# Attention with cluster masks, a routed and a dense expert layer on one core: another order of the opening, of GpSimd's additions and of the seam between the two expert layers

## The reference

```python
# attention: 2 batches, 8 heads, 768 tokens, 64 wide; 16 centroids a head
q_assign = argmax(normed(q) @ normed(centroids).T)      # cluster of each query, the same for k
mask     = q_assign[..., :, None] == k_assign[..., None, :]
scores   = where(mask, (q @ k.T) / sqrt(64), -1e9)
x        = softmax(scores) @ v                          # -> x: 1536 tokens x 512
# routed experts: 8 experts, 512 -> 1024 -> 512, the best one for each token
expert   = argmax(normed(x) @ normed(expert_emb).T / tau)
x        = gate * (relu(x @ w1[expert]) @ w2[expert])   # gate: the softmax at that expert
# dense experts: 8 experts, all of them for each token
P        = exp(x @ w_gate - max)
for _ in range(8):                                      # rows, then columns, brought to a sum
    P /= P.sum(1) ; P /= P.sum(0) ; P *= 1536 / 8
out      = sum(P[:, e] * (relu(x @ w1[e]) @ w2[e]) for e in range(8))
```

## Time and profile before

| | us |
|---|---|
| median of 3 runs | 1592.2 (1591.24 to 1592.25) |
| the profiled execution, its own time | 1594.29 |
| its span in the trace | 1592.5 |
| TensorE busy | 1568.3 (98%) |
| VectorE busy | 1190.0 (75%) |
| ScalarE busy | 770.6 (48%) |
| GpSimd busy | 263.7 (17%) |

### The profile page before, as it was taken

One profiled execution on the slowest core, in us unless ns is written; L12 is line 12 of the kernel. 1 busy time (PEld: TensorE's weight loads), 2 busy tenths in 40 slices (PEclk: granted clock), 3 DMA queues, 4 the chain that ended last, 5 costly groups with the idle time before them and its releaser, 6 DMA issues.

```text
span 1592.5 us, 27473 instructions
## 1 busy us (share of the span) xinstructions
PE 1568.3 (98%) x8404; PEld 1390.7 (87%) x8404; DVE 1190.0 (75%) x2026; ACT 770.6 (48%) x1418; POOL 263.7 (17%) x343
## 2 busy tenths in 40 slices
PE   8999999999999999999999999999999999999998
PEld 7999999778888788989999898989899998989897
DVE  7999999999999976876656666666656566666664
ACT  5777779888888852323232323233232333232321
POOL 2111111342333550000100100010001001100102
PEclk9999999999999999999999999999999999999999
DMA  4222323354344310100110010011001100100002
GB/s 101 61 60 69 79 59 90 86 198 148 143 151 151 106 41 27 40 28 27 47 33 27 29 51 27 27 40 40 27 27 45 35 27 28 52 26 27 27 0 79
DMA packets 123701, 94.92 MB, mean 60 GB/s; under 512 B 66345, under 2 KB 101161, under 8 KB 123633
## 3 DMA queue, kind: packets, MB, share of 16 engines
q1 hardware_dynamic: 120848, 86.01, 17.8%
q0 software_dynamic: 2480, 8.13, 1.5%
q10 hardware_dynamic: 304, 0.05, 0.0%
HBM read 87.88 MB, written 6.29 MB: 59 GB/s over the span
## 4 chain that ended last, share of the span: by engine, by line
PE 88%; DVE 7%; issue 3%; ACT 2%; DVEq 0%; DMA 0%; ACTq 0%; POOL 0%
PE moe_bank L1381 11%; PE moe_bank L1383 11%; PE moe_bank L1382 11%; PE moe_bank L1356 10%; PE moe_bank L1359 10%; PE moe_bank L1358 10%; PE attn_ps_out L447 3%; PE attn_ps_probs_t L428 2%; PE moe_bank L1316 2%; PE moe_bank L1318 2%; PE moe_bank L1317 2%; PE moe_bank L1299 2%; PE moe_bank L1301 2%; PE moe_bank L1300 2%; DVE attn_scores L697 1%
## 5 line engine op out<-in xcount | busy, mean ns | idle before, releaser
L2035 DVE SCALAR_TENSOR_TENSOR all_x<-moe_bank,all_x 128x512 f32<-128x512 f32 x336 | 251.4, 749 | 130.8 <-PE moe_bank L1383 130.2
L1356 PE MATMUL moe_bank<-moe_x_t_hi,all_w_hi 128*128 128x384 f32 x896 | 303.0, 338 | 2.0 <-DVE all_w_lo L889 1.4
L1359 PE MATMUL moe_bank<-moe_x_t_hi,all_w_lo 128*128 128x384 f32 x896 | 302.5, 338 | 0.0
L1381 PE MATMUL moe_bank<-moe_w_hi,moe_h_hi 128*128 128x512 f32 x768 | 302.3, 394 | 0.0
L1358 PE MATMUL moe_bank<-moe_x_t_lo,all_w_hi 128*128 128x384 f32 x896 | 301.1, 336 | 0.0
L1382 PE MATMUL moe_bank<-moe_w_lo,moe_h_hi 128*128 128x512 f32 x768 | 300.5, 391 | 0.0
L1383 PE MATMUL moe_bank<-moe_w_hi,moe_h_lo 128*128 128x512 f32 x672 | 264.5, 394 | 0.0
L1356 PEld LDWEIGHTS moe_bank<-moe_x_t_hi,all_w_hi 128*128 128x128 f32 x896 | 168.4, 188 | 13.4 <-issue 2.0
L1358 PEld LDWEIGHTS moe_bank<-moe_x_t_lo,all_w_hi 128*128 128x128 f32 x896 | 168.4, 188 | 10.0
L1359 PEld LDWEIGHTS moe_bank<-moe_x_t_hi,all_w_lo 128*128 128x128 f32 x896 | 168.2, 188 | 0.0
L2196 POOL TENSOR_TENSOR moe_w_sums<-moe_dense_w_raw 128x256 f32<-128x256 f32 x32 | 24.8, 774 | 842.4 <-DVE all_w_lo L889 842.4
(11 more groups left out here) (339 smaller groups left out, 3071.4 us busy)
## 6 DMA issues: line engine op xcount, KB each, us to landing
...
moe_dense_w_raw<-in_moe_w SPq DMA_DIRECT2D x32, 512.0 KB, 3.4
...
```

What stands on the lines that cost most here:

```text
L1356: pe.matmul(out, hi[:, s, k, :], XH[chunk][:, x, k, :], start=(start and k == 0), stop=False, skip_group_check=True)
L1359: mm = pe.matmul(out, lo[:, s, k, :], XH[chunk][:, x, k, :], start=False, stop=(stop and k == 1), skip_group_check=True)
L1381: pe.matmul(out, HH[h][hidden][:, rows], W2H[j][:, f, :], start=(f == 0), stop=False)
L2035: dve.scalar_tensor_tensor(acc, y, PROB[:, row, bass.ds(at, 1)], acc, ALU.mult, ALU.add).then_inc(y_added, 1)
```

## The change

In the opening, `UnitRows` is now one object for the centroids and one for the embeddings, each with its own load, root and writes. The embeddings are squared and written by ScalarE, and made exact on VectorE behind the splits of head 0. k's first loads go through ScalarE's queue, the embeddings' and tau's through SP's. The centroids' splits stand ahead of those of the second and third thirds; head 0's similarities are computed by thirds, each when its third is split; the first block of scores and four fillers follow them, and the third block of scores now comes ahead of head 1's similarities and the embeddings' transposes. Head 1's third third is transposed behind the key ids and split behind the first two maxima.

In the items the row addition is two operations of 128x256, each of which waits until VectorE has split half of the next item's w2. The token sums of pairs 0, 1 and 2 stand behind the additions of items 13, 14 and 15, with a third buffer; all are GpSimd's. That buffer lies where the dense w1's second landing place is, so `load1(0, 1)` waits until pair 2 is transposed. In the last item VectorE splits the hidden rows ahead of w2's last two parts. In the first unit the sums and splits of the second weight part come earlier on all three engines (ahead of pair 4's sums on GpSimd), and pair 5 is transposed ahead of the fourth chained product.

The diff, cut to what is spoken of, by engine and place:

```diff
-WARM = (8, 4, 6)
+WARM = (8, 4, 4, 6)
...
+    def sums_of_squares(self, act):
+        act.wait_ge(self.loaded, 16)
+        act.activation(self.square[:], self.raw[:], ACT.Square, accum_out=self.s[0]).then_inc(self.summed, 1)
...
+    def write_by_scalar(self, act):
+        act.wait_ge(self.step, self.SCALED)
+        for out, raw in self.outputs():
+            act.activation(out, raw, ACT.Copy, scale=self.s[2]).then_inc(self.written, 1)
```

SP:

```diff
-            for half in range(2):
-                sp.dma_start(KR[0][:, :, half, :], kd[0:1].rearrange("o p t d -> p (o t) d")).then_inc(first_k, 16)
             sp.dma_start(VR[0][:], vd[0:1].rearrange("o p t d -> p (o t) d")).then_inc(first_v, 16)
+            embeddings.load(sp)
             load(1, 1)
+            sp.dma_start(TAU[:, 0:1], tau.rearrange("(o n) -> o n", o=1).broadcast_to([P, 1])).then_inc(tau_loaded, 16)
```

TensorE, opening:

```diff
-            pe.wait_ge(prep_lo, 3)
-            similarities(0, 0, ps_o[:, P:P + 2 * T * NC], 0)
-            similarities(0, 0, ps_o[:, P:P + 2 * T * NC], T).then_inc(prep_ready, 1)
+            for first in range(0, 2 * T, 4):
+                pe.wait_ge(prep_lo, first // 4 + 1)
+                mm = similarities(0, 0, ps_o[:, P:P + 2 * T * NC], first, 4)
+            mm.then_inc(prep_ready, 1)
+            scores(0, 0, 0)
+            warm(WARM[2], ps_s[1][:, 1])
             pe.wait_ge(raw_loaded[1], LOADS)
             transpose_raw(1, 0, 4, ps_s[1][:, 0]).then_inc(prep_ready, 1)
             transpose_raw(1, 4, 4, ps_s[1][:, 1]).then_inc(prep_ready, 1)
-            transpose_raw(1, 8, 4, ps_t[:, 1]).then_inc(prep_ready, 1)
-            scores(0, 0, 0)
             pe.wait_ge(idb_ready, 1)
             key_ids(ps_t[:, 0], 0)
             key_ids(ps_p[:], 3)
+            transpose_raw(1, 8, 4, ps_t[:, 1]).then_inc(prep_ready, 1)
             pe.wait_ge(prep_lo, 5)
             scores(1, 1, 0)
+            pe.wait_ge(max_done, 1)
+            scores(2, 2, 0)
             pe.wait_ge(kid_ready, 2)
             pe.wait_ge(prep_lo, 6)
             similarities(1, 1, ps_p[:], 0)
-            pe.wait_ge(rows.step, rows.DONE)
+            pe.wait_ge(embeddings.written, 2)
...
-            pe.wait_ge(max_done, 1)
-            scores(2, 2, 0)
             for s in range(14):
```

ScalarE, opening:

```diff
-            rows.load(act)
-            act.dma_start(TAU[:, 0:1], tau.rearrange("(o n) -> o n", o=1).broadcast_to([P, 1])).then_inc(tau_loaded, 16)
-            rows.roots(act)
-            act.wait_ge(made, 4)
-            act.activation(TABLE[:], c["rank16"][:, 0:1], ACT.Exp)
+            cents.load(act)
+            for half in range(2):
+                act.dma_start(KR[0][:, :, half, :], kd[0:1].rearrange("o p t d -> p (o t) d")).then_inc(first_k, 16)
+            cents.roots(act)
...
+            embeddings.sums_of_squares(act)
+            embeddings.roots(act)
+            act.wait_ge(made, 4)
+            act.activation(TABLE[:], c["rank16"][:, 0:1], ACT.Exp)
+            embeddings.write_by_scalar(act)
```

The buffers of the token sums:

```diff
+              mem.at("token_sums2", [P, 4, 2 * P], F32, scratch_at)]
+        SUMS_OF_PAIR = [XS[0], XS[1], XS[2], XS[0], XS[1], XS[0]]
```

SP, behind the items:

```diff
             load2(0, 0)
-            load1(0, 1)
             sp.wait_ge(w1_lo, len(W1_PARTS) * ITEMS)
             load2(0, 1)
+            sp.wait_ge(x_t, 4 * GT)
+            load1(0, 1)
```

TensorE, first unit:

```diff
+                transpose_pair(5)
                 pe.wait_ge(copied, 3)
                 multiply(a, 0, 0, A22, T4, False, True).then_inc(chain, 1)
-                transpose_pair(5)
```

ScalarE, first unit:

```diff
                 act.activation(CP1[:], a, ACT.Copy).then_inc(copied, 1)
+                summed_weights(0, 1)
                 hi_parts(3)
```

VectorE, last_tile:

```diff
+                h_part(n, 0)
                 w2_part(n, r, 2)
                 w2_part(n, r, 3)
-                h_part(n, 0)
```

GpSimd, add_rows:

```diff
-                pool.tensor_tensor(OUT[:, bass.ds(t, 1), :].rearrange("p o d -> p (o d)"),
-                                   OUTZ[:, bass.ds(s, 1), :].rearrange("p o d -> p (o d)"), Y[n % 2][:], ALU.add
-                                   ).then_inc(ry_added, 1)
+                for half, (cols, done) in enumerate(((slice(0, D // 2), ry_half), (slice(D // 2, D), ry_added))):
+                    if n + 1 < ITEMS:
+                        pool.wait_ge(rw2_lo, W2_PARTS * (n + 1) + 2 * half + 2)
+                    if half == 1:
+                        pool.wait_ge(ry_half, n + 1)
```

GpSimd, the items' loop and behind it:

```diff
-                if n >= ITEMS - 5 and n < ITEMS - 3:
-                    all_token_sums(n - (ITEMS - 5))
+                if ITEMS - 6 <= n < ITEMS - 3:
+                    token_sums(n - (ITEMS - 6))
             add_rows(ITEMS - 2)
             next_weight_sums()
-            all_token_sums(2)
-            all_token_sums(3)
-            all_token_sums(4)
+            token_sums(3)
+            weight_sums(0, 1)
+            token_sums(4)
             add_rows(ITEMS - 1)
             token_sums(5)
-            weight_sums(0, 1)
```

131 lines of the change are left out of this document (59 added, 72 removed).

## The result

The changed kernel takes **1615.12 us** (median of 4 runs, 1613.64 to 1616.01) against 1592.22 (4 runs, 1591.24 to 1592.50): the ratio is 1.0144, 95% interval 1.0129 to 1.0159, 22.9 us slower. The forecast was 1591.8 with 1588.2 to 1596.3. The profiled execution took 1615.6 us, its span is 1613.8, 21.3 more than the span before.

A forecast was written before the change was run, and what follows sets the result against it. TensorE, busy 98% of the span, was taken as the bound. Opening −0.9, items +0.1 and seam 1.2 made 0.4 us gained: 1593.9 for the profiled execution, 1591.8 for the median standing 2.1 lower, range 1588.2 to 1596.3.

The forecast's parts named there:

- Step (1): Opening, the centroids' chain: TensorE can begin the similarities at about 8.2 us instead of 10.14.
- Step (2): Opening, head 0's 24 similarity matmuls: 4.4 us where the clock falls on the way, ending at 12.6.
- Step (3): Opening, reduction to first mask: 4.05 us instead of 4.75, mask at 15.15, or 16.85 after one fall, against 19.56.
- Step (4): Opening: VectorE waits for the embeddings' transposes, third maximum at 21.3 to 24.05; 0.9 us lost, bounds 2.1 gained, 2.9 lost.
- the second fall: Opening's first steps at half clock: reduction at 26.1 to 27.0 instead of 25.59; lasting longer was a rival, chance 0.13.
- the rule on transposes: Last item: transposes don't count as clock activity, so the clock would fall there as before; part of a rival, chance 0.10.
- the tie of which the rival speaks: Items: if VectorE's w1 split starts just before a GpSimd sum, that sum waits behind the 2.3 us split.
- frame of item 14: Items, times with TensorE starting item 14 at 495.7: item 16's gather starts at 509.8, lands at 514.0, wanted at 514.06.
- gathers come late: Items: a lost tie makes TensorE wait 4.0 us for gathered rows; one gives 1595.8, two 1598.0; chance 0.20.
- 2.25 gained forecast: Last item: hidden rows split earlier, no 1.90 us wait or clock fall, first unit at 565.0 against 567.26.
- 0.95 of those 2.25 given back: Seam: later weight load and sums melt the gain; unit 1's second product at 581.5 against 582.84, 1.3 us gained.
- Both signs under which I was to be wrong: Unit 1's second product over 2.5 us earlier relative to item 13, or the third maximum before 21.5.

The follow-up runs named there:

- e13: The whole changed kernel with four, two and five fillers put into the opening's three TensorE waits: 1608.95 us against 1593.44 for the kernel before.
- e14: The changed kernel with the old order of first steps and seam, gathers issued earlier, four fillers before the second block of scores: 1597.41 us against 1593.44 before.
- e1: The kernel before with the change of attention's opening alone: 1600.02 us against 1593.20.
- e7: The kernel before with seven more fillers (11 instead of 4) ahead of head 0's similarities: 1592.38 us against 1592.67.
- e3: The kernel before with one edit, the hidden rows' first half split ahead of w2's last two parts in the last item: 1592.66 us against 1593.20.
- e17: e7 with a filler ahead of every fourth of the 24 thin matmuls, and with e3's edit: 1592.99 us, ratio 0.9999 to the kernel before.
- e2: The kernel before with the change of the items, the last item and the seam alone: 1605.11 us against 1593.20.
- e4: e2 with the gather of an item's rows issued ahead of the addition and sums on GpSimd's queue: 1596.39 us, 8.7 us faster than e2.
- e9: e2 with the row addition in one operation that doesn't wait for VectorE: 1596.18 us against 1593.12 for the kernel before.
- e15: The same kernel as e1, on another chip: 1602.54 us against 1593.44 for the kernel before.

## Why the prediction was wrong

**The bound** was read rightly: what VectorE got back in twelve items moved nothing. The direction was wrong, in three terms of the sum: the price of the four sums and the landing ahead of a gather (11.1 us lost where 0.1 was to be gained), the way from the similarities to the third maximum with the length of the fall behind it (8.2 where 0.9 was to be lost), and the price of the weight sums behind the late load (4.7 where 0.95 was to be lost).

**The opening: 0.9 lost forecast, 8.2 in the trace.** Step (1) was 1.5 us too optimistic (similarities at 9.66 against 8.2): q's first rows landed later, and TensorE's transposes of q and k took 0.21 us each, where they had taken 0.12, though the table of stretches has full clock there. Step (2) met its end (12.45 against 12.6) by luck: it counted a fall in the similarities, and they ran at full clock from a later start. Step (3) failed: the mask stood at 18.50 against 16.85. I counted 4.05 us from the reduction and left out that head 1's transposes now stand behind a block of scores and four fillers, which run at 0.43 us each after the fall; VectorE waited 2.64 us for them. Step (4) named the right wait and its place, and the third maximum came at 26.33 against 22.85 to 24.05.

The largest error is the length of the second fall. I took the reduction 0.5 to 1.4 us late and bounded the opening at 2.9; the one fall that the rows let me measure had lasted some 6.7 us. Here it lasted 13.7 us, worth 6 us by e13, and the reduction came 5.4 us late. Against the rule on transposes I had weighed one row, the clock's return at 17.6. The Trainium skill ("TensorE: Matmul & The Clock Gate", Part 4: PE-mode transpose) says that transposes don't count as activity. The stretch from 22.8 to 36.4, with transposes, thin matmuls and two blocks of scores ahead of the fillers, and e14's 10.2 us are what the rule would lead one to expect; e1, whose clock came back at 28.1 in the same stretch, speaks against it, and no run here tells the two sorts of matmul apart.

**The gathers: 0.1 gained forecast, 11.1 lost with what follows.** The term that failed is the price of the four sums: 0.7 + 1.72 + 0.7 + 1.6 = 4.7 us, where they took 8.0 (1.78, 1.77, 2.79, 1.60). I had taken 0.7 for two sums as beside a split from PSUM. But the 0.73 of the earlier trace rows is no row for that: it is the sum that began 0.05 us ahead of a split from SBUF, the tie of which the rival speaks. Here the first sum began 0.04 us behind one. And 1.72 was not the worst, as 2.79 shows. The landing took 6.6 us, the value of a gather beside a weight load, where I used 4.2. In the frame of item 14 (times less the 7.7 us by which item 15 is late) the gather thus started at 513.2 instead of 509.8. The rival "gathers come late" named this mechanism and priced one at 4.0 us (5.5 measured, 3.1 for the other), without the slow clock behind it; it had a chance of 0.20, two of them reached only 1598.0 beside an opening that lost 0.9 (the second priced at 2.2 without a working), and the range left two out.

**The last item: 2.25 gained forecast, 2.16 measured, by luck.** 1.2 us of it is the fall of the clock that the trace of before happened to have; e7 hasn't it with the same code. The edit alone is worth nothing that can be measured (e3 and e17). The other 1.0 us comes with the halves of the addition: e2, e4 and the changed kernel need 13.6 us there, e3, e9 and e17, where the addition is in one piece, 14.6.

**The seam: 0.95 of those 2.25 given back forecast, 4.7 lost from the first unit to the second layer.** Last item and seam together were to gain 1.3 (the sum enters 1.2, a slip) and lost 2.5. The wait of `summed_weights` for GpSimd's sums was in the working, with 569.6 for pair 3's splits; they came at 590.66, or 571.9 when the 18.8 us are taken off by which the last item is late. The load landed 0.8 to 1.2 us later than I took, the four weight sums took 4.5 us instead of 3.2, and behind them come 2.25 us of waiting at pair 4 and a fall of the clock. e4 loses 3.7 us here at full clock, so the fall is the smaller part.

What was right: splits of w2 at 1.18 us each in the plain items, the wait of VectorE before the logits' columns (1.5 or more said, 3.09 found), half clock between 17 and 25 us, no fall at 557 in the last item, and the sums of pair 4 behind the summed weights. Both signs under which I was to be wrong looked to the fast side; none looked to the side on which it failed.

What stays open: the medians of the whole lose 21.6 to 22.9 us, those of the parts 18.7 to 21.0, and the spans add up with e15's opening and not with e1's. That points to the falls. Why the changed kernel fell into the long one in both of its profiles, and kept its runs within 2.4 us, while the same opening alone had a short one in e1, isn't settled.
